# Moving the flags of the second routing's counts to the stationary side, with 16-bit digits and a state per token

## The chip, the cores and the metric

One NeuronCore of a Trainium2 chip runs the whole program. The metric is the device time in microseconds (us) of one execution. In the rows, PE is TensorE's matmuls, PEld its loads of the stationary operand, DVE is VectorE, ACT is ScalarE, POOL is GpSimd, and SP is SyncE, which issues transfers.

## The reference

The program computes attention, then a mixture of experts with free routing (MoE 1), then a second one with limited places (MoE 2). The change lies mostly in MoE 2:

```python
def _moe2_ref(x, w_gate, w1, w2):
    N, D = x.shape            # 3072, 512
    E = w_gate.shape[1]       # 8; w1[e] is 512 x 1024, w2[e] 1024 x 512
    cap = N // E              # 384 places per expert
    flat = (x @ w_gate).flatten()
    order = np.argsort(-flat)
    assigned = -np.ones(N); counts = np.zeros(E)
    for idx in order:                        # best score first
        tok, e = idx // E, idx % E
        if assigned[tok] >= 0 or counts[e] >= cap:
            continue
        assigned[tok] = e; counts[e] += 1
    ...
    for e in range(E):
        h = np.maximum(x[assigned == e] @ w1[e], 0.0)
        out[assigned == e] = h @ w2[e]
```

## The kernel before

The kernel has three stages in time: attention to about 225 us, MoE 1 to about 389 us, MoE 2 to the end. Tokens lie as 128 partitions by NT = 24 columns.

**MoE 1** runs 10 tiles of 128 tokens. In each, TensorE makes the hidden layer in two halves (L1017), ScalarE applies the relu to each half (L1289), and TensorE multiplies by the second matrix (L1032) once both halves are there.

**MoE 2, the routing.** The greedy loop of the reference is replaced by E - 1 = 7 phases and a last list. A phase k takes each free token's best open expert (`first_best`, L1460 to L1464, the best score in `value`, the expert as a one-hot `cand_h`) and finds the score at which the first expert is full. It finds that score's 32 bits in six rounds of 4, 4, 6, 6, 6 and 6 bits. A round r has 15 or 63 candidate digits, made into float thresholds by integer operations on `key`. VectorE compares all values with them into `reach` (L1672, two halves of 12 columns). TensorE counts per expert and threshold (L1065, 24 matmuls with `cand_h[:, j, :]`, 8 columns, stationary and 63 flags moving). VectorE compares the counts with the room left (L1682), TensorE spreads the flags over the partitions (L1070), VectorE counts the flags to get the digit (L1686) and updates `key`. Then follow ties, the list of the tokens and its transfer (L1074, L1049, L1050, L1085). In all a phase has 16 TensorE steps, numbered n = 0 to 15: 2r and 2r+1 are the two of round r, 12 is L1074, 13 and 14 are L1049 with L1050 (12 after the sums of L1708, 13 and 14 after the scans of L1610), 15 is L1085 (one-hot rows made by L1629).

**MoE 2, the experts.** TensorE, expert by expert: 32 "up" products (L1124, 8 blocks f of 4; the trace shows each product as two instructions), relu of each block on ScalarE (L1309), and 24 "down" products (L1137, 3 row blocks c of 8). The steps of the routing are written between these products by `expert2`: `product(units)` adds 3 for an up product and 4 for a down product, and step n is written when the sum reaches its number in `spacing`. While expert i runs, the steps AHEAD to 15 of phase i+1 come first, and then the steps 0 to AHEAD-1 of phase i+2. Steps 0 to 15 of phase 0 and 0 to AHEAD-1 of phase 1 run before the first expert, when TensorE has nothing else. After 18 of the 24 down products `turn2` transposes the next expert's tokens (L1097), which POOL has gathered by indirect transfers (L810) from the list.

```python
            AHEAD = 4
            UP, DOWN = 3, 4
            TURN_AT = CT * FC - 6
            spacing = [18, 7, 8, 7] + [12, 8] * (ROUNDS - 2) + [15, 11, 8, 17]
```

Order is set by these hand-written queues and by semaphores; `plink` makes each dependent VectorE instruction wait for the one before.

## Time and profile before

| | us |
|---|---|
| median of 3 runs | 870.46 (867.44 to 872.6) |
| the profiled execution's own time | 868.02 |
| its span, first to last instruction | 865.7 |
| TensorE busy in the span | 756.2 (87%) |
| VectorE busy | 375.1 (43%) |

The profiled execution's time is 2.3 us above its span, and 2.4 us below the median of the runs. The page cuts the span into 40 slices, and gives the busy share in each and the granted clock of TensorE, whose two levels are 1.2 and 2.4 GHz.

### The profile page before, as it was taken

What the parts mean: (1) busy time and instruction counts of PE and PEld (TensorE: products, weight loads), DVE (VectorE), ACT (ScalarE), POOL (GpSimd) and SP (SyncE); (2) the same over time, 40 slices, a digit from 0 to 9 for tenths busy, and PEclk for the clock granted to TensorE, in tenths of its full rate; (3) what the DMA queues carried; (4) which work ended last, traced back from release to release, by engine and by line L of the source; (5) the groups of instructions that cost most, each with busy time, mean ns of one, the idle gap of its engine ahead of it and who ended that gap; (6) DMA issues with size and microseconds to landing.
All of it is one profiled execution on the core that took longest, in us unless ns stands there. A gap on an engine that the chain in (4) does not pass through costs nothing.

```text
span 865.7 us, 14421 instructions
## 1 busy us (share of the span) xinstructions
PE 756.2 (87%) x4750; PEld 514.1 (59%) x4750; DVE 375.1 (43%) x1532; ACT 221.0 (26%) x685; POOL 189.9 (22%) x251
## 2 busy tenths in 40 slices
PE   3888989995699999992269999999999999999996
PEld 2788989995568778661135454454544545445552
DVE  3576777786111121125735537355473554700000
ACT  3667787881001111110011111111101111011110
POOL 8364646440111111111010200202002020121101
PEclk9799999996699999995559999999999999999998
DMA  9899986687743369000240703306042060453000
GB/s 222 183 196 218 214 204 148 154 245 281 271 165 109 138 221 390 21 4 6 93 140 0 256 14 142 126 0 256 12 159 109 0 257 13 173 190 137 37 0 37
DMA packets 130468, 119.91 MB, mean 139 GB/s; under 512 B 95858, under 2 KB 95858, under 8 KB 130224
## 3 DMA queue, kind: packets, MB, share of 16 engines
q1 hardware_dynamic: 118192, 88.45, 33.9%
q10 hardware_dynamic: 6464, 14.73, 5.5%
q0 software_dynamic: 5760, 16.03, 5.1%
q8 instruction: 33, 0.54, 0.3%
q14 instruction: 19, 0.16, 0.1%
HBM read 105.95 MB, written 16.50 MB: 141 GB/s over the span
## 4 chain that ended last, share of the span: by engine, by line
PE 76%; DVE 10%; issue 5%; DMA 3%; SPq 3%; ACT 1%; POOL 1%; ACTq 0%; POOLq 0%; another core or an unknown queue 0%; DVEq 0%
PE bank L1124 21%; PE bank L1137 18%; PE bank L1017 9%; PE bank L1032 8%; PE bank L1065 4%; PE bank L877 3%; PE bank L898 3%; PE bank L920 2%; PE bank L887 1%; SPq L466 1%; PE bank L1097 1%; DVE scratch L1347 1%; PE bank L997 1%; DVE shared L1358 1%; PE bank L1070 1%
## 5 line engine op out<-in xcount | busy, mean ns | idle before, releaser
L1124 PE MATMUL bank<-scratch,weights 128*128 128x384 f32 x512 | 182.3, 501 | 0.7 <-ACT scratch L1303 0.7
L1137 PE MATMUL bank<-weights,scratch 128*128 128x512 f32 x384 | 176.9, 604 | 4.9 <-issue 2.5
L1124 PEld LDWEIGHTS bank<-scratch,weights 128*128 128x128 f32 x512 | 94.1, 191 | 61.5 <-issue 5.2
L1137 PEld LDWEIGHTS bank<-weights,scratch 128*128 128x128 f32 x384 | 68.5, 190 | 74.5 <-issue 72.0
L1206 ACT ACTIVATE scratch<-shared,neg_max 128x120 f32<-128x120 f32 x192 | 73.4, 383 | 33.5 <-DVE neg_max L1358 20.9
L1309 ACT ACTIVATE scratch<-bank 128x384 f32<-128x384 f32 x64 | 31.5, 492 | 169.9 <-PE bank L1124 169.9
L665 POOL TENSOR_TENSOR scratch<-scratch,row_inv 128x480 f32<-128x480 f32 x48 | 47.4, 988 | 79.8 <-DVE row_inv L1368 79.6
L1017 PEld LDWEIGHTS bank<-mix,weights 128*128 128x128 f32 x512 | 61.2, 197 | 5.1 <-issue 5.1
L1017 PE MATMUL bank<-mix,weights 128*128 128x128 f32 x512 | 62.1, 280 | 1.4 <-DVE mix L1572 1.4
L807 POOL COPY idx<-token_list 128x3 int32 (+1 forms) x8 | 1.5, 186 | 263.6 <-DVE token_list L1645 257.2
L1032 PE MATMUL bank<-weights,mix 128*128 128x512 f32 x128 | 58.4, 599 | 0.0
L1315 ACT COPY scratch<-bank 128x512 f32<-128x512 f32 x24 | 14.1, 587 | 165.0 <-PE bank L1137 165.0
L877 PE MATMUL bank<-scratch 128*128 128x120 f32 x384 | 54.3, 288 | 2.0 <-POOL scratch L657 2.0
L1358 DVE CUSTOM_DVE_ANT_0 shared<-bank,scratch 128x120 f32<-128x120 f32 x192 | 42.7, 279 | 29.4 <-PE bank L877 29.3
L1672 DVE TENSOR_TENSOR mix<-mix 128x756 bf16<-128x756 f32 (+1 forms) x70 | 54.7, 823 | 1.2
L898 PE MATMUL bank<-shared,mix 120*128 120x128 f32 x384 | 51.2, 276 | 4.2 <-issue 2.3
L822 POOL DMA_INDIRECT out<-scratch,idx x24 | 23.8, 990 | 138.3 <-ACT scratch L1315 136.5
L1065 PEld LDWEIGHTS bank<-mix 128*8 128x8 bf16 x1008 | 32.9, 88 | 31.5 <-DVE mix L1672 27.5
L877 PEld LDWEIGHTS bank<-scratch 128*128 128x128 f32 x384 | 48.9, 200 | 2.4 <-POOL scratch L657 2.4
L898 PEld LDWEIGHTS bank<-shared,mix 120*128 120x128 f32 x384 | 47.1, 193 | 4.7 <-issue 2.5
L1065 PE MATMUL bank<-mix 128*8 128x63 bf16 (+1 forms) x1008 | 39.1, 190 | 12.2 <-DVE mix L1672 12.0
L1682 DVE TENSOR_SCALAR mix<-bank,mix 8x63 bf16<-8x63 f32 (+1 forms) x42 | 10.8, 257 | 72.6 <-PE bank L1065 70.6
(230 smaller groups left out, 950.4 us busy)
## 6 DMA issues: line engine op xcount, KB each, us to landing
weights<-in_moe_w SPq DMA_DIRECT2D x20, 2048.0 KB, 8.0
scratch<-in_moe_w SPq DMA_DIRECT2D x8, 2048.0 KB, 15.8
weights<-in_moe_w ACTq DMA_DIRECT2D x16, 512.0 KB, 6.2
mix<-in_v SPq DMA_DIRECT2D x40, 192.0 KB
rows<-row SPq DMA_DIRECT2D x24, 264.5 KB, 3.5
weights<-in_k SPq DMA_DIRECT2D x24, 256.0 KB, 4.9
scratch<-in_q SPq DMA_DIRECT2D x24, 256.0 KB, 4.3
weights<-in_v ACTq DMA_DIRECT2D x24, 192.0 KB, 3.9
```

The lines of the kernel that those rows point to most:

```text
L665: nc.gpsimd.tensor_tensor(out=x, in0=x, in1=inv, op=ALU.mult).then_inc(s.p_scaled, 1)
L877: last = mm(sc[g % 2][:, h * W:(h + 1) * W], qbd[g // 2 % 2][:, h, g % 2, :], kwin[b % 2][:, h, n, :], start=True, stop=True)
L898: last = mm(ob[g % 2][:, h * P:(h + 1) * P], vwin[g % VR][0:W, h * P:(h + 1) * P], pT[g % 2][0:W, h * P:(h + 1) * P], start=True, stop=True)
L1017: last = mm(o, w1_sb[at_][:, c, f * P:(f + 1) * P], xT1[:, c, :], start=(c == 0), stop=(c == C - 1), skip_group_check=True)
L1032: last = mm(yb[:, :], hT1[:, f, :], w2_sb[at_][:, f, :], start=(f == 0), stop=(f == FC - 1))
L1065: last = mm(counts[0:E, 0:ROUND_KEYS[r]], cand_h[:, j, :], reach[:, j, 0:ROUND_KEYS[r]], start=(j == 0), stop=(j == NT - 1), skip_group_ch ...
L1124: last = mm(hb2[f % 2][:, 0:CAP], w1_sb[odd][:, c, f * P:(f + 1) * P], xT2[odd][:, c, :], start=(c == 0), stop=(c == C - 1), skip_group_ch ...
L1137: last = mm(yb2[c % 2][:, :], hT2[odd][:, f, c * P:(c + 1) * P], w2_sb[odd][:, f, :], start=(f == 0), stop=(f == FC - 1), skip_group_check ...
L1206: a.activation(probs[g % PR][:, h, :], masked[g % 2][:, h, :], ACT.Exp, bias=neg_max[:, g % 2, h:h + 1], scale=-1.0, accum_out=row_sum[:, ...
L1309: a.activation(hT2[odd][:, f, :], bank[3 + f % 2][:, 0:CAP], ACT.Relu).then_inc(s.hidden2_s, 1)
L1358: v_.tensor_tensor_reduce(masked[g % 2][:, h, :], bank[g % 2][:, h * W:(h + 1) * W], m, -SCALE, FAR, ALU.add, ALU.min, neg_max[:, g % 2, h ...
L1672: v_.tensor_tensor(out=reach[:, a_:b_, 0:wide_r], in0=value[:, a_:b_].rearrange("p (j o) -> p j o", o=1).to_broadcast(shape), in1=keys.bit ...
```

## The change

The counts change sides: `reach`, the flags of 15 or 63 keys, becomes the stationary operand and `cand_h` with 8 columns the moving one, so that the counts lie as keys by experts. The room of each expert can then be compared in place (the matmul L1063, its semaphore `told` and a copy go), and the sum step spreads 8 columns instead of 63. The key is no longer built as a number: after round 0 each token's score is cut into six digits in 16-bit floats, and a `state_h` per token holds its next digit, or something beyond the range if the token has already fallen above or below. Rounds 1 to 5 compare that state with a constant row of keys, both 16-bit, in pairs of columns. AHEAD becomes 6. The wait for the relu is split, in MoE 2 (the eighth block is awaited only before the eighth product) and in MoE 1 (the second half before the fifth). A few copies of 8 columns become an addition of 0.0.

```diff
-        reach = apart(NT, KEYS, dt=BF16)
-        thresholds = apart(KEYS, dt=I32)
-        key = apart(1, dt=I32)
-        sign = apart(1, dt=I32)
+        reach = apart(NT // 2, KEYS, 2, dt=BF16)
+        sign_i = apart(NT, dt=I32)
+        order_i = apart(NT, dt=I32)
+        digits_i = apart(len(BITS), NT, dt=I32)
+        digits_h = apart(len(BITS), NT, dt=BF16)
+        state_h = apart(NT, dt=BF16)
+        alive_h = apart(NT, dt=BF16)
+        past_h = apart(NT, dt=BF16)
         digit = apart(1)
-        digit_i = apart(1, dt=I32)
-        enough = apart(KEYS)
-        enough_h = apart(KEYS + 1, dt=BF16)
-        remain_col = apart(1)
+        enough_h = apart(E, dt=BF16)
         above = apart(2 * NT, dt=BF16)
         both_n = apart(2 * E, dt=BF16)
...
-                const(nc.gpsimd.iota(digit_row[:, :], pattern=[[1, KEYS]], base=1, channel_multiplier=0))
+                const(nc.gpsimd.iota(digit_row[:, :], pattern=[[1, ROUND_KEYS[0]]], base=1, channel_multiplier=0))
+                const(nc.gpsimd.iota(iota_keys[:, :, :], pattern=[[1, KEYS], [0, 2]], base=1, channel_multiplier=0,
+                                     allow_small_or_imprecise_dtypes=True))
...
-                        pe.wait_ge(s.hidden_made, CREDIT + 2 * g + 2)
+                        pe.wait_ge(s.hidden_made, CREDIT + 2 * g + 1)
                         for f in range(FC):
+                            if f == FC // 2:
+                                pe.wait_ge(s.hidden_made, CREDIT + 2 * g + 2)
                             if f == FC - 2:
                                 pe.wait_ge(s.gathered, 16 * (g + 2))
                                 turn1()
...
                             pe.wait_ge(s.judged, 3 * ROUNDS * k + 3 * r + 1 + j // (NT // 2))
-                        if n == 0 and j == 0:
-                            pe.sem_inc(s.waits_apart, 1)
-
-                            mm(tot[0:E, 0:1], room_e[0:1, :], ones_f[0:1, 0:1], start=True, stop=True,
-                               skip_group_check=True).then_inc(s.told, 1)
-                        last = mm(counts[0:E, 0:ROUND_KEYS[r]], cand_h[:, j, :], reach[:, j, 0:ROUND_KEYS[r]],
+                        last = mm(counts[0:ROUND_KEYS[r], 0:E], reach[:, j // 2, 0:ROUND_KEYS[r], j % 2], cand_h[:, j, :],
                                   start=(j == 0), stop=(j == NT - 1), skip_group_check=True)
                     last.then_inc(s.counted, 1)
                 elif n < 2 * ROUNDS:
                     pe.wait_ge(s.judged, 3 * ROUNDS * k + 3 * r + 3)
-                    mm(counts[:, 64:64 + ROUND_KEYS[r]], ones[0:E, :], enough_h[0:E, 0:ROUND_KEYS[r]], start=True, stop=True,
+                    mm(counts[:, 64:64 + E], ones[0:ROUND_KEYS[r], :], enough_h[0:ROUND_KEYS[r], :], start=True, stop=True,
...
-            AHEAD = 4
+            AHEAD = 6
...
             spacing = [18, 7, 8, 7] + [12, 8] * (ROUNDS - 2) + [15, 11, 8, 17]
...
-                pe.wait_ge(s.hidden2_s, CREDIT + FC * (i + 1))
+                pe.wait_ge(s.hidden2_s, CREDIT + FC * i + FC - 1)
                 for c in range(CT):
 
                     pe.wait_ge(s.y2_s, CREDIT + CT * i + (1 if c == 2 else 0))
                     for f in range(FC):
+                        if c == 0 and f == FC - 1:
+                            pe.wait_ge(s.hidden2_s, CREDIT + FC * (i + 1))
...
                 lg = bank[7][:, 0:NL]
-                v_.tensor_copy(row[t % 2][:, 0:E], lg[:, 0:E])
+                v_.tensor_scalar(row[t % 2][:, 0:E], lg[:, 0:E], 0.0, None, ALU.add)
...
-                link(v_.tensor_scalar(digits_at[r], digit_row[:, 0:ROUND_KEYS[r]], SHIFTS[r], None, ALU.logical_shift_left))
-
+            link(v_.tensor_scalar(first_digits[:, :], digit_row[:, :], SHIFTS[0], None, ALU.logical_shift_left))
             half = ROUND_KEYS[0] // 2
-            v_.tensor_scalar(first_keys[:, 0:half], digits_at[0][:, 0:half], -1, None, ALU.bitwise_xor)
-            link(v_.tensor_scalar(first_keys[:, half:], digits_at[0][:, half:], -(1 << 31), None, ALU.bitwise_xor))
+            v_.tensor_scalar(first_keys[:, 0:half], first_digits[:, 0:half], -1, None, ALU.bitwise_xor)
+            link(v_.tensor_scalar(first_keys[:, half:], first_digits[:, half:], -(1 << 31), None, ALU.bitwise_xor))
             dve.wait_ge(s.scores_in, 16)
 
             ROUNDS = len(BITS)
@@ -1658,47 +1655,47 @@
                 first_best(plink, scores2, value, hot, cand_h)
                 for r in range(ROUNDS):
                     wide_r = ROUND_KEYS[r]
-                    flags = counts[:, 64:64 + wide_r]
-                    keys = first_keys[:, :] if r == 0 else thresholds[:, 0:wide_r]
-                    if r == 1:
-                        plink(v_.tensor_scalar(keys, digits_at[r], key, None, ALU.bitwise_xor))
-                    elif r:
-
-                        plink(v_.tensor_scalar(keys, digits_at[r], key, digit_i, ALU.bitwise_xor,
-                                               ALU.bitwise_xor))
-
-                    for a_, b_ in ((0, NT // 2), (NT // 2, NT)):
-                        shape = [P, b_ - a_, wide_r]
-                        v_.tensor_tensor(out=reach[:, a_:b_, 0:wide_r],
-                                         in0=value[:, a_:b_].rearrange("p (j o) -> p j o", o=1).to_broadcast(shape),
-                                         in1=keys.bitcast(F32).rearrange("p (o k) -> p o k", o=1).to_broadcast(shape),
-                                         op=ALU.is_ge).then_inc(s.judged, 1)
+                    state = digits_h[:, 0, :] if r == 0 else state_h
+                    for a_, b_ in ((0, NT // 4), (NT // 4, NT // 2)):
+                        shape = [P, b_ - a_, wide_r, 2]
+                        if r == 0:
+                            ins = v_.tensor_tensor(
+                                out=reach[:, a_:b_, 0:wide_r, :],
+                                in0=value[:, 2 * a_:2 * b_].rearrange("p (j o s) -> p j o s", o=1, s=2).to_broadcast(shape),
+                                in1=first_keys[:, :].bitcast(F32).rearrange("p (o k u) -> p o k u", o=1, u=1).to_broadcast(shape),
+                                op=ALU.is_ge)
+                        else:
+                            ins = v_.tensor_tensor(
+                                out=reach[:, a_:b_, 0:wide_r, :],
+                                in0=iota_keys[:, 0:wide_r, :].rearrange("p (o k) s -> p o k s", o=1).to_broadcast(shape),
+                                in1=state[:, 2 * a_:2 * b_].rearrange("p (j o s) -> p j o s", o=1, s=2).to_broadcast(shape),
+                                op=ALU.is_le)
+                        ins.then_inc(s.judged, 1)
                     if r == 0:
-                        dve.wait_ge(s.told, ph + 1)
-                        plink(v_.tensor_copy(remain_col[0:E], tot[0:E, 0:1]))
-                    elif r > 1:
-                        plink(v_.tensor_tensor(out=key, in0=key, in1=digit_i, op=ALU.bitwise_xor))
+                        plink(v_.tensor_scalar(sign_i, value.bitcast(I32), 31, -(1 << 31), ALU.arith_shift_right,
+                                               ALU.bitwise_or))
+                        plink(v_.tensor_tensor(out=order_i, in0=value.bitcast(I32), in1=sign_i, op=ALU.bitwise_xor))
+                        for i in range(ROUNDS):
+                            ins = v_.tensor_scalar(digits_i[:, i, :], order_i, SHIFTS[i], ROUND_KEYS[i],
+                                                   ALU.logical_shift_right, ALU.bitwise_and)
+                        plink(ins)
+                        v_.tensor_copy(digits_h[:, 0, :], digits_i[:, 0, :])
+                        plink(v_.tensor_scalar(digits_h[:, 1:, :], digits_i[:, 1:, :], 1.0, None, ALU.add))
                     dve.wait_ge(s.counted, 2 * ROUNDS * ph + 2 * r + 1)
-                    v_.tensor_scalar(enough_h[0:E, 0:wide_r], counts[0:E, 0:wide_r], remain_col[0:E], None,
-                                     ALU.is_ge).then_inc(s.judged, 1)
+                    v_.tensor_tensor(out=enough_h[0:wide_r, :], in0=counts[0:wide_r, 0:E], in1=room_e[0:wide_r, :],
+                                     op=ALU.is_ge).then_inc(s.judged, 1)
                     dve.wait_ge(s.counted, 2 * ROUNDS * ph + 2 * r + 2)
-
-                    plink(v_.tensor_scalar(enough[:, 0:wide_r], flags, 0.5, 0.0, ALU.is_gt, ALU.add, accum_out=digit))
-                    shift = SHIFTS[r]
-                    if r == 0:
-                        plink(v_.tensor_copy(digit_i, digit))
-                        plink(v_.tensor_scalar(key, digit_i, shift, None, ALU.logical_shift_left))
-                        plink(v_.tensor_scalar(sign, key, 31, -1, ALU.arith_shift_right, ALU.bitwise_xor))
-                        plink(v_.tensor_scalar(sign, sign, -(1 << 31), None, ALU.bitwise_or))
-                        plink(v_.tensor_tensor(out=key, in0=key, in1=sign, op=ALU.bitwise_xor))
-                    else:
-                        plink(v_.tensor_scalar(digit_i, digit, float(1 << shift), None, ALU.mult))
-                plink(v_.tensor_tensor(out=key, in0=key, in1=digit_i, op=ALU.bitwise_xor))
-
-                closing = key.bitcast(F32)
-                v_.tensor_scalar(above[:, 0:NT], value, closing, None, ALU.is_gt)
-                v_.tensor_scalar(above[:, NT:], value, closing, None, ALU.is_ge)
-                plink(v_.tensor_scalar(equal_t, value, closing, None, ALU.is_equal))
+                    plink(v_.tensor_reduce(digit, counts[:, 64:64 + E], AX, ALU.max))
```

The first place is TensorE's queue at the end of an expert's up products and the start of its down products (`product` steps 12 to 15). Before:

```order
L1124 MATMUL bank<-scratch,weights 128x384 x3
L1073 ISA
L1074 MATMUL bank<-mix,ones 128x16 [waits totals_done]
L1130 ISA [waits w2_in0]
L1133 ISA [waits hidden2_s]
L1137 MATMUL bank<-weights,scratch 128x512 [waits y2_s]
L1137 MATMUL bank<-weights,scratch 128x512 x2
L1077 REGISTER_ALU
L1049 MATMUL bank<-mix,before 128x24 [waits totals_done]
L1050 MATMUL bank<-mix,ones 128x23
L1137 MATMUL bank<-weights,scratch 128x512 x2
L1049 MATMUL bank<-mix,before 128x24 [waits mine_ready]
```

And now (line numbers of the changed kernel; L1121 is the up product, L1136 the down product):

```order
L1071 MATMUL bank<-mix,ones 128x16 [waits totals_done]
L1121 MATMUL bank<-scratch,weights 128x384 x3
L1119 REGISTER_ALU
L1121 MATMUL bank<-scratch,weights 128x384 [waits hidden2_s]
L1074 REGISTER_ALU
L1051 MATMUL bank<-mix,before 128x24 [waits totals_done]
L1052 MATMUL bank<-mix,ones 128x23
L1121 MATMUL bank<-scratch,weights 128x384 x3
L1051 MATMUL bank<-mix,before 128x24 [waits mine_ready]
L1052 MATMUL bank<-mix,ones 128x23
L1127 REGISTER_ALU [waits w2_in1]
L1136 MATMUL bank<-weights,scratch 128x512 [waits y2_s,hidden2_s]
```

Steps 12, 13 and 14 now stand among the up products; the wait of `hidden2_s` at the first L1136 is for seven blocks, that for the eighth comes later (not shown). Between step 12 and the second L1051 stand 7 up products; before it was 5 down products and the full relu wait.

The second place is TensorE's queue in front of the first expert (steps of phase 1, then `turn2`). Before:

```order
L1085 MATMUL bank<-mix 128x6 x24
L1063 MATMUL bank<-ones_f,mix 8x1
L1065 MATMUL bank<-mix 8x15 x24
L1070 MATMUL bank<-mix,ones 128x15
L1065 MATMUL bank<-mix 8x15 x24
L1070 MATMUL bank<-mix,ones 128x15
L1097 MATMUL bank<-ident,scratch 128x128 x12
```

And now:

```order
L1082 MATMUL bank<-mix 128x6 x24
L1062 MATMUL bank<-mix 15x8 x24
L1067 MATMUL bank<-mix,ones 128x8
L1062 MATMUL bank<-mix 15x8 x24
L1067 MATMUL bank<-mix,ones 128x8
L1062 MATMUL bank<-mix 63x8 x24
L1067 MATMUL bank<-mix,ones 128x8
L1094 MATMUL bank<-ident,scratch 128x128 x12
```

A third round of phase 1, the first with 63 keys, has moved in front of the first expert.

## Rows read from the trace of the kernel before

**Rows 1.** The page's head: span, busy time of each engine.
```profile
span 865.7 us, 14421 instructions
PE 756.2 (87%) x4750; PEld 514.1 (59%) x4750; DVE 375.1 (43%) x1532; ACT 221.0 (26%) x685; POOL 189.9 (22%) x251
```
**Rows 2.** Windows: stretch, its us, busy by engine, clock, DMA.
```profile
390.00:442.00 52.00, 12.68 (x232) 9.65 (x232) 33.30 (x126) 0.00 (x0) 5.54 (x7) 0.50 0.21 59
500.00:740.00 240.00, 234.07 (x1381) 123.19 (x1380) 118.95 (x424) 32.98 (x63) 26.09 (x29) 1.00 0.26 98
```
**Rows 3.** Timeline of PE in the second expert: start, us, what.
```profile
508.12 2.85 PE L1124 MATMUL bank<-scratch,weights 128*128 128x384 f32 x8
510.90 0.92 PE L1065 MATMUL bank<-mix 128*8 128x63 bf16 x24
511.74 2.20 PE L1124 MATMUL bank<-scratch,weights 128*128 128x384 f32 x6
513.88 0.20 PE L1070 MATMUL bank<-mix,ones 8*128 8x63 bf16 x1
514.01 2.85 PE L1124 MATMUL bank<-scratch,weights 128*128 128x384 f32 x8
```
**Rows 4.** The same timeline, from up to down products.
```profile
528.49 0.17 PE L1074 MATMUL bank<-mix,ones 128*128 128x16 bf16 x1
529.24 2.84 PE L1137 MATMUL bank<-weights,scratch 128*128 128x512 f32 x6 [0.57 <-ACT scratch L1309]
533.77 0.18 PE L1049 MATMUL bank<-mix,before 128*128 128x24 bf16 x1
```
**Rows 5.** Timeline of PE, last expert, which has no steps.
```profile
814.84 20.86 PE L1124 MATMUL bank<-scratch,weights 128*128 128x384 f32 x64
836.32 20.84 PE L1137 MATMUL bank<-weights,scratch 128*128 128x512 f32 x48 [0.63 <-issue]
```
**Rows 6.** Timeline of DVE after step 12 of that phase.
```profile
528.73 0.17 DVE L1714 TENSOR_TENSOR mix<-mix,bank 128x8 f32<-128x8 f32 x1 [0.82 <-PE bank L1074]
533.38 0.21 DVE L1610 TENSOR_TENSOR_SCAN mix<-mix 128x24 bf16<-128x24 bf16 x1
```
**Rows 7.** Timeline of PE: 8 moving columns in MoE 1.
```profile
298.27 0.96 PE L997 MATMUL bank<-gate_weights,mix 128*128 128x8 f32 x8
299.12 5.42 PE L1032 MATMUL bank<-weights,mix 128*128 128x512 f32 x12
```
**Rows 8.** Timeline of PE, end of the sixth expert.
```profile
752.08 0.78 PE L1085 MATMUL bank<-mix 128*128 128x6 bf16 x24
752.72 1.96 PE L1137 MATMUL bank<-weights,scratch 128*128 128x512 f32 x4
759.72 2.82 PE L1137 MATMUL bank<-weights,scratch 128*128 128x512 f32 x6
763.93 1.09 PE L1097 MATMUL bank<-ident,scratch 128*128 128x128 f32 x8 [1.39 <-DMA scratch<-rows,idx]
```
**Rows 9.** Timeline of PE, rounds 0 and 1 of phase 2.
```profile
491.17 0.18 PE L1070 MATMUL bank<-mix,ones 8*128 8x15 bf16 x1 [0.44 <-issue]
493.44 0.75 PE L1065 MATMUL bank<-mix 128*8 128x15 bf16 x24 [0.18 <-DVE mix L1672]
```
**Rows 10.** Timeline of DVE, phase 0, a 63-key round and L1629.
```profile
404.68 1.80 DVE L1672 TENSOR_TENSOR mix<-mix 128x756 bf16<-128x756 f32 x2
407.38 0.27 DVE L1682 TENSOR_SCALAR mix<-bank,mix 8x63 bf16<-8x63 f32 x1 [0.83 <-PE bank L1065]
408.78 1.80 DVE L1672 TENSOR_TENSOR mix<-mix 128x756 bf16<-128x756 f32 x2
429.19 1.76 DVE L1629 TENSOR_TENSOR mix<-iota_pair,mix 128x3072 bf16<-128x3072 bf16 x1
```
**Rows 11.** Timeline of PE at the lower clock, phases 0 and 1.
```profile
431.50 0.88 PE L1085 MATMUL bank<-mix 128*128 128x6 bf16 x24 [3.14 <-DVE mix L1638]
442.16 2.91 PE L1097 MATMUL bank<-ident,scratch 128*128 128x128 f32 x12
```

25 lines of the change are left out of this document (15 added, 10 removed).

## Prediction, made before the changed kernel ran

> **What bounds the kernel now.** I began with the page's head: TensorE is busy for 756 of 866 us [rows 1]. The windows show where it is not. From 500 to 740 us it is busy 234 of 240 us at the full clock, VectorE only half [rows 2]: there every instruction put into TensorE's queue costs its time, and VectorE's work costs nothing unless TensorE arrives before it. From 390 to 442 us it is the other way round: TensorE is busy 12.7 of 52 us at 1.2 GHz, VectorE 33 [rows 2]. So I price the change twice: by TensorE's queue in the loops, by the length of the dependent chain in front of the first expert. Attention and MoE 1 hardly move: in MoE 1 the down products follow at once on the 8 gate matmuls [rows 7], so the split wait there removes nothing, and I take it at 0.
>
> **The relu wait.** Step 12 starts at 528.49, the first down product at 529.24, and the page names the relu [rows 4]. Without the wait L1074 would hold the queue for some 0.05, so 0.7 is saved in each of six experts. In the last one 64 up instructions take 20.86 with a tail of 0.49, a pitch of 0.323; the down products could start at 835.53 and do at 836.32: 0.8, in two experts [rows 5]. Block seven is done long before, block eight (0.5 of relu) has seven products of 0.85 as cover. Sum -5.8.
>
> What is late next is VectorE. It needs from step 12 (528.49) to the end of its second scan (533.38 + 0.21) 5.1, with 0.05 for the signal 5.15 [rows 4, 6]. Before, TensorE reached the second L1049 at 5.28 after step 12, just behind. Now seven up products (7 x 0.647 = 4.53) and two or three insertions (0.13 each; eight up instructions before L1065 take 2.78 in place of 2.59 [rows 3]) make 4.8. TensorE waits 0.35 at step 14, in six experts: +2.1. Queued behind it are the expert's down products, which ScalarE's copies and POOL's scatters then get later. Step 15 then has four products (3.4) against VectorE's unchanged 3.3, as before.
>
> **The counts.** 24 of them, 8 columns stationary and 63 moving, hold the queue from 510.90 to 511.74, 0.84 [rows 3]. After it 63 columns are stationary and 8 move. The trace has no such load; the bounds are two rows with 128 stationary columns. The 32-bit ones of L997, 8 columns moving, take 299.12 - 298.27 = 0.85 for 8, 0.106 each, 0.83 ns a column [rows 7]; 63 columns by that are 0.052, 24 of them 1.26, with 0.1 for handing over to the next product 1.35: +0.5 a round. The 16-bit ones of L1085 take 752.72 - 752.08 = 0.64 for 24 [rows 8]: -0.2 a round. I take the first. Half the bytes of L997's would make L1085's loads twice as quick; they are four times as quick, 0.21 ns a column. So something beyond width helps the full 128 columns of 16 bits, and nothing in the trace says that 63 columns have it. This is where I chose, and it decides the case. 23 rounds of 63 keys remain among the products (24 before: four each in phases 1 to 6): +11.5. Rounds of 15 keys have loads of 0.0125 by either price, under their pitch of some 0.03: no change.
>
> The Trainium skill, TensorE: Matmul & The Clock Gate, section Weight-path perf modes — Fast Weight Load (FWL) and DoubleRow, says that the fast load is on only with exactly 128 weights and a type other than fp32. By its section on LDWEIGHTS a plain load takes the columns over 1.2, 52.5 ns for 63. The trace's two rates fit it (0.106 and 0.027 for 128 columns); that it holds for 63 no row shows. By the rule the counts cost what I take, by L1085's row 16 us less.
>
> **The sum step** moves 8 in place of 63 columns: at 2.4 GHz 0.023 less, 23 times, -0.5. **The moved round.** One full round (count and sum step) leaves the queue of the loops: 514.01 - 508.12 less 14 x 0.323, 1.4: -1.4. **Waits in rounds 0 and 1.** At round 1 TensorE waits 0.18 for the flags [rows 9]; VectorE's key update and threshold (five small operations) shrink to three, with two products as cover: gone, five times, -0.9. The 0.44 before round 0's sum step [rows 9] I leave as it is: L1063 goes, but six digits and their conversion come before VectorE's comparison, about 1.5 by the rows of small operations (0.2 a dependent link). Bounds: -2.2, and +2 if that chain ends after the counts.
>
> **The last gather.** In the sixth expert TensorE could turn at 759.72 + 6 x 0.427 = 762.3 and does at 763.93, waiting for the gather [rows 8]. The list is now written 20 units, five down products or 4.3, earlier: -1.6. The gather of expert 1 before the loop is hidden too.
>
> **In front of the first expert.** A 63-key round takes 408.78 - 404.68 = 4.10: 2.70 from flags to comparison, 1.40 from there to the next flags [rows 10]. The 16-bit flags in pairs run like L1629, 3072 elements in 1.76 [rows 10], so 756 in about 0.55 in place of 0.9; TensorE can start at 0.6 and needs 1.35 and its end: 2.2 in place of 2.7. The second part stays about 1.35, three links on 24 columns in place of threshold and key. With the lost key operations at the end phase 0 is 2.8 shorter, and so are the list and the gather; phase 1's own rounds give 0.2. But the third round of phase 1 now stands before `turn2`, at 442.16 until now [rows 11]: 1.0 to make the state, 2.2, 0.3 for the sum step: +3.5. Net +0.5. The round no longer hides behind up products there.
>
> The small copies turned additions and the set-up (one shift for six) lie beside transfers: 0.
>
> **Sum:** -5.8 + 2.1 + 11.5 - 0.5 - 1.4 - 0.9 - 1.6 + 0.5 = +3.9 on the profiled 868.0: 871.9. The median of the runs shown is 2.4 higher, so 874.
>
> **Rivals.**
> *Cheap loads* (chance 0.15). 63 columns load at L1085's rate. Then counts give 23 x -0.2 = -4.6, and each of the five serial rounds is 0.65 shorter, -2.8 in place of +0.5 at the start: -15.5, 855. For it: L1085 reads the same 16-bit layout, with a step of two. Against it: the reasons above. The skill's rule speaks against it.
> *Half-hidden loads* (0.13). A load overlaps more with the array's work, pitch about 0.045: +0.25 a round: 23 x 0.25 = 5.8 in place of 11.5, start -0.5: -2.8, 867.5. For it: in rows 3 all of a count's 8-column load is already out of sight.
> *Slower by the lower clock* (0.12). The loads before the first expert might take twice as long at 1.2 GHz: 2.5 in place of 1.26 for a count, in five serial rounds (four of phase 0, one of phase 1): +6.2, 880.5. It decides from 0.055 us a load up. Against it: L1085 takes 0.88 there and 0.64 at the full clock [rows 8, 11], 1.4 times, not 2.
> *My forecast* (0.6), own range 869 to 879, from +0.3 to +0.6 a count and the bounds of round 0.
>
> **Chances.** A measurement of this kernel can tell about 0.5%, 4.4 us. My forecast lies at +3.9, so of its 0.6 I give 0.36 to no change and 0.24 to slower; cheap loads are faster; half-hidden ones are split evenly; the lower clock is slower. Faster 0.15 + 0.07 = 0.22, same 0.36 + 0.06 = 0.42, slower 0.24 + 0.12 = 0.36. The range 862 to 880 leaves out cheap loads and the end of the last rival.
>
> **What would show it.** In the profile after: L1062 with 63 keys, 24 of them from first start to the next product 1.35 (cheap: 0.65); no ACT wait before the first L1136, but some 0.35 before the second L1051; an expert with its steps about 1.4 longer than before; `turn2`'s first L1094 near 442.7 with no gather wait; no wait for the gather in the sixth expert; the flags on VectorE at 0.55. Wrong would make me above all the price of a 63-column load; next a VectorE chain in round 0 that ends after the counts, or a wait at step 14 larger than reckoned.

## The result, and the profile after

The changed kernel takes 867.0 us (median of 20 runs, 858.9 to 871.5) where the kernel before takes 871.2 (20 runs, 867.1 to 875.3). The ratio is 0.9948, with a 95% interval of 0.9927 to 0.9969: about 3 to 6 us faster. I had forecast 874, no change or slower. The span of the profiled execution falls from 865.7 to 860.1, its own time from 868.0 to 865.4: after the change 5.3 lie outside the span, where 2.3 did before. Most other executions have 2.3, and nothing in the profile tells where the rest went. Two executions of later runs, of 2672 and 1571 us where the others of their kernels took about 855 and 859, are left out of medians and ratios; what held them up isn't known.

The profiled execution of the changed kernel is shorter than most. The 20 runs have spans from 856.6 to 869.2 with a median of 864.6, and mean granted clocks from 0.946 to 0.933 with a median of 0.9375; the longer ones tend to have the lower clock. The profiled one has 860.1 and 0.942. The granted clock has two levels, so these numbers give some 108 us at 1.2 GHz for the median run and 100 for the profiled one. By my estimate that is worth up to 4 of the 4.5 us between them, half of the 8, as far as TensorE is the bound in those stretches. The run with four steps ahead, below, shows where such a stretch can lie.

The head of the page after and its row of the granted clock, then the windows that answer to [rows 2]:

```profile
span 860.1 us, 14325 instructions
PE 752.6 (88%) x4736; PEld 516.2 (60%) x4736; DVE 347.3 (40%) x1513; ACT 220.9 (26%) x685; POOL 190.6 (22%) x251
...
PEclk9799999997699999996569999999999999999999
```
```profile
390.00:442.00 52.00, 13.05 (x241) 11.17 (x242) 30.98 (x136) 0.00 (x1) 5.65 (x8) 0.52 0.22 62
500.00:740.00 240.00, 233.21 (x1353) 124.07 (x1353) 102.79 (x425) 33.43 (x64) 26.43 (x29) 1.00 0.26 98
```

Over the whole span VectorE has lost 28 us of work and TensorE 3.6. In the loops TensorE is the bound as before: 233 of 240 us.

The timeline of TensorE in the second expert answers to [rows 3] and [rows 4]: start, us, what, and in brackets the idle time and who ended it.

```profile
501.10 2.75 PE L1121 MATMUL bank<-scratch,weights 128*128 128x384 f32 x8
503.78 0.94 PE L1062 MATMUL bank<-mix 128*63 128x8 bf16 x24
504.65 2.21 PE L1121 MATMUL bank<-scratch,weights 128*128 128x384 f32 x6
506.80 0.18 PE L1067 MATMUL bank<-mix,ones 63*128 63x8 bf16 x1
506.90 2.85 PE L1121 MATMUL bank<-scratch,weights 128*128 128x384 f32 x8
...
526.52 0.19 PE L1051 MATMUL bank<-mix,before 128*128 128x24 bf16 x1 [0.20 <-DVE mix L1607]
526.56 0.17 PE L1052 MATMUL bank<-mix,ones 128*128 128x23 bf16 x1
526.73 3.67 PE L1136 MATMUL bank<-weights,scratch 128*128 128x512 f32 x8
```

Four things can be read here. 24 counts hold TensorE's queue from 503.78 to 504.65: 0.87, where they held it 0.84 before [rows 3]. I had forecast 1.35. The sum step holds it 0.10 in place of 0.13. The first down product no longer waits for ScalarE [rows 4]. Step 14 waits 0.20 for VectorE. An expert with its steps takes 53.85 in place of 53.67, where I had said about 1.4 longer.

Round 0 of the next phase, on all three engines (it answers to [rows 9], one phase on). POOL's L810 issues the gathers of the next expert's rows, L822 a scatter of results:

```profile
534.12 0.60 DVE L1662 TENSOR_TENSOR mix<-mix,first_keys 128x180 bf16<-128x180 f32 x2
535.07 0.59 DVE L1679 TENSOR_SCALAR mix<-mix 128x24 int32<-128x24 int32 x6
535.77 0.21 DVE L1683 TENSOR_SCALAR mix<-mix 128x120 bf16<-128x120 int32 x1
538.21 0.15 DVE L1685 TENSOR_TENSOR mix<-bank,mix 15x8 bf16<-15x8 f32 x1 [2.22 <-remote]
...
535.34 0.75 PE L1062 MATMUL bank<-mix 128*15 128x8 bf16 x24
536.02 1.13 PE L1136 MATMUL bank<-weights,scratch 128*128 128x512 f32 x2
538.42 0.17 PE L1067 MATMUL bank<-mix,ones 15*128 15x8 bf16 x1 [1.27 <-issue]
...
534.55 1.05 POOL L810 DMA_INDIRECT scratch<-rows,idx  x1 [0.31 <-issue]
535.91 1.00 POOL L810 DMA_INDIRECT scratch<-rows,idx  x1 [0.30 <-issue]
537.21 1.01 POOL L822 DMA_INDIRECT out<-scratch,idx  x1 [0.30 <-issue]
```

VectorE's digits end at 535.98 and the last count starts at 535.93, but the comparison of the counts starts only at 538.21, 2.3 later. TensorE then waits 1.27 before the sum step, where it waited 0.44 before. In the rounds after this one the comparison comes 0.20 behind the last count. The trace also has the time of the semaphore's update, the signal itself: it comes 2.25 behind the start of the last count, and the comparison starts 0.03 after it. In the rounds after this one it comes after 0.18 or 0.19. So VectorE is not what is late. It is the signal, or the counts behind it, since the profile only models the ends of matmuls. There is a new cost of 0.8 in five phases that no term of my sum has.

The sixth expert (against [rows 8]) no longer waits for its gather, and waits 0.77 for VectorE once, as before:

```profile
748.88 0.19 PE L1051 MATMUL bank<-mix,before 128*128 128x24 bf16 x1 [0.77 <-DVE mix L1607]
...
753.10 7.11 PE L1136 MATMUL bank<-weights,scratch 128*128 128x512 f32 x16
760.05 1.04 PE L1094 MATMUL bank<-ident,scratch 128*128 128x128 f32 x8
```

A 63-key round of phase 0 on VectorE and TensorE (against [rows 10]) takes 410.32 - 406.95 = 3.37 in place of 4.10. The flags take 1.01 for both halves and 24 counts at 1.2 GHz 1.45. In round 0 of that phase the comparison starts 1.01 behind the last count, where it started 0.21 behind it before: the digits stand ahead of it and nothing covers them. No term of my sum has that either.

```profile
406.95 1.01 DVE L1668 TENSOR_TENSOR mix<-iota_keys,mix 128x756 bf16<-128x756 bf16 x2
409.04 0.16 DVE L1685 TENSOR_TENSOR mix<-bank,mix 63x8 bf16<-63x8 f32 x1 [1.08 <-PE bank L1062]
410.32 1.02 DVE L1668 TENSOR_TENSOR mix<-iota_keys,mix 128x756 bf16<-128x756 bf16 x2
...
407.56 1.45 PE L1062 MATMUL bank<-mix 128*63 128x8 bf16 x24 [1.49 <-DVE mix L1668]
```

Where the time went, from the starts of single instructions (an expert runs from its first up product to the next one's). The last two columns are profiles of the same two kernels on another chip, which come in below:

```
                                  before   after  | before   after (chip D)
start of VectorE's phase 0        396.93  399.35  | 400.88  400.68
from there to the first expert     48.81   47.86  |  47.68   47.08
first expert                       56.58   53.89  |  55.04   54.81
second to fifth expert            214.72  215.37  | 211.73  210.08
sixth                              53.85   50.50  |  52.24   50.50
seventh                            43.93   43.06  |  43.93   43.06
eighth, to the end                 50.90   50.04  |  50.90   50.04
```

Two of these rows are no effect of the change. The 2.4 ahead of phase 0 come with attention: MoE 1's first hidden product already starts at 225.03 before and 227.66 after. In the first expert the clock rises to 2.4 GHz at 451.5 before, 5.8 into the expert, and at 447.0 after, at its start; on chip D it rises at 452.5 before and 452.2 after, and the expert differs by 0.23. The rest of the gain is in the last three experts. The four in the middle, which carry 16 of the 23 rounds of 63 keys, lose 0.65 here and gain 1.65 on chip D.

### The profile page after: what moved, and what is told of

Its sections match the earlier page's. It is cut to its first block, busy times and chain, and to the rows that moved or that the text cites. A ratio compares the mean times of both kernels' runs of the same rounds, so it can differ in the third digit from the quotient of the medians.

```text
span 860.1 us, 14325 instructions
## 1 busy us (share of the span) xinstructions
PE 752.6 (88%) x4736; PEld 516.2 (60%) x4736; DVE 347.3 (40%) x1513; ACT 220.9 (26%) x685; POOL 190.6 (22%) x251
## 4 chain that ended last, share of the span: by engine, by line
PE 73%; DVE 13%; issue 4%; SPq 3%; DMA 2%; POOL 1%; ACT 1%; ACTq 0%; another core or an unknown queue 0%; POOLq 0%; DVEq 0%
PE bank L1136 18%; PE bank L1121 17%; PE bank L1017 9%; PE bank L1034 8%; PE bank L1062 4%; PE bank L877 3%; PE bank L898 3%; PE bank L920 2%; PE bank L887 2%; SPq L465 1%; PE bank L1094 1%; DVE scratch L1346 1%; PE bank L997 1%; DVE shared L1357 1%; PE bank L864 1%
## 5 line engine op out<-in xcount | busy, mean ns | idle before, releaser
L1121 PE MATMUL bank<-scratch,weights 128*128 128x384 f32 x512 | 178.0, 495 | 0.7 <-ACT scratch L1302 0.7
L1136 PE MATMUL bank<-weights,scratch 128*128 128x512 f32 x384 | 177.7, 603 | 0.0
L1121 PEld LDWEIGHTS bank<-scratch,weights 128*128 128x128 f32 x512 | 93.0, 189 | 60.0 <-issue 4.7
L1136 PEld LDWEIGHTS bank<-weights,scratch 128*128 128x128 f32 x384 | 68.8, 190 | 67.9 <-issue 66.5
L1062 PEld LDWEIGHTS bank<-mix 128*63 128x63 bf16 (+1 forms) x1008 | 35.6, 110 | 46.3 <-DVE mix L1662 18.5
L822 POOL DMA_INDIRECT out<-scratch,idx x24 | 23.7, 989 | 169.9 <-ACT scratch L1314 168.1
L1062 PE MATMUL bank<-mix 128*63 128x8 bf16 (+1 forms) x1008 | 39.4, 174 | 24.3 <-DVE mix L1662 14.5
L1685 DVE TENSOR_TENSOR mix<-bank,mix 63x8 bf16<-63x8 f32 (+1 forms) x42 | 6.6, 156 | 90.4 <-PE bank L1062 78.5
L1034 PEld LDWEIGHTS bank<-weights,mix 128*128 128x128 f32 x128 | 23.1, 190 | 23.0 <-issue 23.0
```

The source lines that it names most:

```text
L822: nc.gpsimd.indirect_dma_start(out=out, out_offset=bass.IndirectOffsetOnAxis(ap=idx2[odd][:, c:c + 1].bitcast(U32), axis=0), in_=y2[odd][: ...
L1034: last = mm(yb[:, :], hT1[:, f, :], w2_sb[at_][:, f, :], start=(f == 0), stop=(f == FC - 1))
L1062: last = mm(counts[0:ROUND_KEYS[r], 0:E], reach[:, j // 2, 0:ROUND_KEYS[r], j % 2], cand_h[:, j, :], start=(j == 0), stop=(j == NT - 1), s ...
L1121: last = mm(hb2[f % 2][:, 0:CAP], w1_sb[odd][:, c, f * P:(f + 1) * P], xT2[odd][:, c, :], start=(c == 0), stop=(c == C - 1), skip_group_ch ...
L1136: last = mm(yb2[c % 2][:, :], hT2[odd][:, f, c * P:(c + 1) * P], w2_sb[odd][:, f, :], start=(f == 0), stop=(f == FC - 1), skip_group_check ...
```

## The experiments

The chips are called A (first four kernels), B, C and D. Each ratio is against the kernel before on the same chip.

**What each part gives** (chip A, before 868.0). The changed kernel itself was not run unaltered on chips A, B and C, so where a run is set against it, that is its profile or its ratio from the result.

The waits alone (in MoE 1 the second half of the relu is awaited singly as well):
```diff
-pe.wait_ge(s.hidden2_s, CREDIT + FC * (i + 1))
+pe.wait_ge(s.hidden2_s, CREDIT + FC * i + FC - 1)
 ...
+    if c == 0 and f == FC - 1:
+        pe.wait_ge(s.hidden2_s, CREDIT + FC * (i + 1))
```


> The kernel before with nothing but the relu waits split (the last relu block awaited singly, in MoE 1 the second half singly). Theory A (the relu wait is what the change gains, and the counts with 63 stationary columns cost about nothing): 0.7 to 0.8 saved in eight experts, 0.2 to 0.35 given back at step 14 in six, so -4 to -5 us against before, ratio 0.9945 to 0.9955, as fast as the whole change. Rival B (the gain is VectorE's shorter chain, and a late VectorE takes over whatever the relu wait leaves): within 1.5 us of before.

Measured 866.0, ratio 0.997 (0.9946 to 0.9993): -2.0 by the medians, -2.6 by the ratio, between the two. The two last experts gave 0.87 each. In an expert with steps the period went from 53.67 to 53.54, because step 14 took up most of what the relu left:

```profile
589.27 0.19 PE L1051 MATMUL bank<-mix,before 128*128 128x24 bf16 x1 [0.45 <-DVE mix L1614]
```

The digits alone (AHEAD = 4 and the old waits in the changed kernel).


> The changed kernel with the old relu waits and four steps ahead: only the digits, the state and the flags as weights are left of the change. Theory A: the counts give +0.7 in all, the sum step -0.5, round 1 -0.9, phase 0 about -3, and the sum step of round 0, which in the changed kernel waits 1.27 in place of 0.45, +4 over five phases: the sum is within 1.5 us of before, 870 to 872.5. Rival B: faster than before by 3 to 5 us, since the gain lies here. My forecast on record, were its price of the loads right: +8 to +11 us.

867.5, ratio 0.9984 (0.996 to 1.0007), within 1 us of before; by the forecast's price of the loads it would have been at 876 to 879. The period was 54.05, with the relu wait of 0.57 to 0.65 and one of 1.17 to 1.24 in round 0.

```diff
-AHEAD = 6
+AHEAD = 4
```


> The changed kernel with four steps ahead in place of six, all else kept. Theory A: the round that leaves the queue of the loops (-1.4) and the gather of the last expert (-1.4) come back, the third round of phase 1 before the first expert (3.2 to 3.5 at the lower clock) goes: within 1 us of the changed kernel. Rival C (the earlier list and gather are the gain of the change): 3 us or more slower than the changed kernel.

866.6, ratio 0.9974 (0.9947 to 1.0). From VectorE's phase 0 to the first expert it took 44.45 in place of 47.86, the sixth expert 52.13 in place of 50.50. So six steps ahead cost 3.4 in front of the first expert, at the lower clock, and return 1.6 in the sixth; between four and six the median can't tell. By the ratios the waits alone give 0.3%, the digits alone 0.2% with 1 in the interval, and the whole change gave 0.5%: no single part carries the gain.

This profile shows something else. Twice, at 545.7 and at 654.9, the granted clock falls to 1.2 GHz among the experts, and is back at 549.1 and 658.3. These two experts take 55.32 and 55.30, the one between them 53.96. The fall comes 0.6 after the end of round 0's wait:

```profile
545.10 0.17 PE L1067 MATMUL bank<-mix,ones 15*128 15x8 bf16 x1 [1.25 <-DVE mix L1685]
545.20 3.32 PE L1136 MATMUL bank<-weights,scratch 128*128 128x512 f32 x4
```
```profile
545.80:549.00 3.20, 3.20 (x26) 1.18 (x25) 0.70 (x4) 0.59 (x1) 0.65 (x1) 0.50 0.26 104
```

The same is in two profiles of chip B: in that of the single loads, whose kernel is the changed one up to its end, at 596.0 and 705.3 (those experts take 55.53, their neighbours 53.87 and 53.80), and in that with POOL held, at 699.8, in the one expert of the last with a wait of 1.13. All five falls begin within 0.7 of the end of a round 0 wait of 1.1 to 1.3; of the 19 waits that long in the profiles, 14 have none behind them. No profile of the kernel before or of its variants, and none on chips C and D, has one among the experts. So a late signal may cost 1.3 to 1.7 beyond its wait, which the profile after, without such a fall, doesn't show. That the wait brings the fall about, and that the lower mean clocks among the 20 runs come from such falls, no run tested.

The kernel before with `AHEAD = 6`.


> The kernel before with six steps ahead and nothing else. Theory A: -1.4 for the moved round, -1.6 for the last gather, and +4.1 for a serial 63-key round of the old kind before the first expert: +1, 871 to 873. Rival C: faster than before by 3 us or more.

874.2, ratio 1.0065 (1.0038 to 1.0092): +6, more than either. With the old 4.1 round the chain ahead of the first expert grows by 4.0, the period by 0.4 (round 0's wait becomes 0.91, and step 14 waits 0.20 with 0.25 of the relu left behind it), and the sixth expert returns 3.3. That makes 2.4 with the four experts in the middle; phase 0 also started 3.2 later in this profile than in that of the kernel before, which is no effect of the edit, and the rest of the 6 I can't place. With the old round six ahead loses 6; with the new one the medians show no loss.

**What a load costs.** Behind the last down product of the changed kernel 24 matmuls of each kind ran, back to back (chip B).
```diff
+for w in (8, 15, 32, 48, 63, 64, 96, 127, 128):
+    for _ in range(24):
+        mm(bank[3][0:w, 0:8], ones[:, 0:w], cand_h[:, 0, :], start=True, stop=True)
 ... (stationary columns with a step of two; 8 with 15, 63, 126 moving; 32 bits)
```


> The changed kernel with extra matmuls behind the last down product, 24 back to back of each kind: 8, 15, 32, 48, 63, 64, 96, 127 and 128 stationary columns of 16 bits with 8 moving; 15, 32 and 63 stationary columns taken with a step of two; 8 stationary columns with 15, 63 and 126 moving; 8, 32, 63 and 128 stationary columns of 32 bits with 8 moving. My forecast on record: 0.052 each for 63 columns of 16 bits, 0.106 for 128 of 32 bits, 0.027 for 128 of 16. Theory L (from the changed kernel's rows): 0.030 to 0.036 for 63 columns of 16 bits whatever the step, near 0.03 for all narrower ones, and growing above 64 if the fast load needs all 128 columns, staying near 0.03 if it doesn't.

Windows of it: us, matmuls (about five of them already under way at the left edge), loads, other engines, and the granted clock as the third number from the end. In order: 63 and 64 columns; 64; 127; 128; then 32-bit, 32 columns and 128 columns.

```profile
861.30:862.20 0.90, 0.90 (x33) 0.90 (x32) 0.00 (x0) 0.00 (x0) 0.00 (x0) 1.00 0.74 291
862.35:862.85 0.50, 0.50 (x14) 0.50 (x12) 0.00 (x0) 0.00 (x0) 0.00 (x0) 0.50 0.15 33
865.10:867.30 2.20, 2.20 (x23) 2.20 (x22) 0.00 (x0) 0.00 (x0) 0.00 (x0) 0.50 0.00 0
867.55:868.15 0.60, 0.60 (x25) 0.60 (x25) 0.00 (x0) 0.00 (x0) 0.00 (x0) 0.50 0.00 0
876.60:877.60 1.00, 1.00 (x37) 1.00 (x35) 0.00 (x0) 0.00 (x0) 0.00 (x0) 1.00 0.00 0
883.00:892.00 9.00, 9.00 (x44) 9.00 (x43) 0.00 (x0) 0.00 (x0) 0.00 (x0) 0.50 0.00 0
```

The clock fell to 1.2 GHz at 862.3, in the middle of the kinds. From start to start, by the single records (the profile has two instructions for each 32-bit matmul, and these are times of one instruction; the 106 at 2.4 GHz is that of rows 7):

```
stationary columns, type      2.4 GHz   1.2 GHz
8 to 48,  16 bits               25 ns
63 or 64, 16 bits               32        53    (63 taken with a step of two: 54)
96        16 bits                         81
127       16 bits                        107
128       16 bits                         27
8 / 32    32 bits               25 / 32
63        32 bits               58       107
128       32 bits    106 [rows 7]        213
8, with 63 / 126 moving, 16 bits          52 / 104
```

Beyond 48 columns, a column of 16 bits costs 0.5 ns at the full clock (63 and 64 columns; wider ones ran only at the lower clock) and 0.84 at the lower one; of 32 bits 0.8 to 0.9 and 1.7. My 0.83 was the 32-bit price at the full clock. The type alone makes most of the factor of two that I had written down and set aside: 1.8 for 63 columns at the full clock (58 against 32), 2.0 at the lower one (107 against 53).

In place, each 63-key count issued twice (chip C, the same edit in both kernels):
```diff
+for twice in range(2 if r > 1 else 1):
     last = mm(counts[...], ...)
```


> The kernel before with each of the 24 count matmuls of every 63-key round issued twice (the first time into columns that nobody reads). It prices a count of the old form (8 stationary columns of 16 bits, 63 moving) in place: 24 rounds of 63 keys run among the products, four in front of the first expert. Expected 24 times about 0.033, 0.8 a round, so +3.2 an expert where TensorE is the bound and about +22 us in all.

> The changed kernel with each count of every 63-key round issued twice in the same way: the price of the new form (63 stationary columns, 8 moving) in place. The price of my forecast on record, 0.052 each: 1.25 a round, +5 an expert. The price that the run of single loads gave at the full clock, 0.032: 0.77 a round, +3.1 an expert, within 0.1 of the old form. So the difference of the two doubled kernels tells what the change of sides costs a round: +0.5 by the forecast, 0.0 by the loads.

Ratios 1.0236 (1.0208 to 1.0263) and 1.0206 (1.0177 to 1.0236). 48 counts of the old form, then of the new:

```profile
565.85 1.62 PE L1066 MATMUL bank<-mix 128*8 128x63 bf16 x48
567.39 2.21 PE L1126 MATMUL bank<-scratch,weights 128*128 128x384 f32 x6
```
```profile
572.33 1.73 PE L1063 MATMUL bank<-mix 128*63 128x8 bf16 x48
574.00 2.21 PE L1123 MATMUL bank<-scratch,weights 128*128 128x384 f32 x6
```

The 24 further ones cost 1.54 - 0.84 = 0.70 and 1.67 - 0.87 = 0.80, 29 and 33 ns each. At the full clock the change of sides costs +0.03 to +0.10 a round, not +0.5.

**The late signal of round 0** (chip B, before 869.8).

POOL holds its gathers until round 0 is counted, in the first four experts:
```diff
+if held:
+    wait_apart(pool, s.counted, 2 * ROUNDS * (e + 1) + 1)
 for c in range(CT):
     nc.gpsimd.indirect_dma_start(
```


> The changed kernel, but GpSimd starts the three gathers of an expert's rows only after TensorE has signalled the 24 counts of round 0 of the running phase (in four experts of the loop; the last two as they were). Theory P (the signal of the counts arrives late because GpSimd is issuing gathers at the time: it comes 2.2 after the last count with gathers beside it, 0.2 in rounds without): VectorE's comparison comes within 0.3 of the counts, TensorE's wait of 1.2 before the sum step of round 0 is gone in those experts, the gather is still in time, so -3 to -5 us against the changed kernel. Rival D (the comparison is late for VectorE's digits or for something on TensorE itself): the wait stays at 1.2, the time is the changed kernel's.

859.4, ratio 0.988 (0.9849 to 0.9911), the period 52.54. The comparison came at 539.68, 0.2 behind the last count, and the wait was gone. In round 1, beside which the gathers now ran, it came 1.65 late, where more products cover it:

```profile
538.89 0.75 PE L1066 MATMUL bank<-mix 128*15 128x8 bf16 x24
539.68 0.15 DVE L1689 TENSOR_TENSOR mix<-bank,mix 15x8 bf16<-15x8 f32 x1
...
541.92 1.05 POOL L812 DMA_INDIRECT scratch<-rows,idx  x1 [0.31 <-issue]
542.65 0.75 PE L1066 MATMUL bank<-mix 128*15 128x8 bf16 x24
543.27 1.00 POOL L812 DMA_INDIRECT scratch<-rows,idx  x1 [0.31 <-issue]
544.89 0.15 DVE L1689 TENSOR_TENSOR mix<-bank,mix 15x8 bf16<-15x8 f32 x1 [2.64 <-PE bank L1066]
545.25 0.17 PE L1071 MATMUL bank<-mix,ones 15*128 15x8 bf16 x1
```

The digits behind the comparison:
```diff
                     ins.then_inc(s.judged, 1)
-                    if r == 0: ... (sign, order, digits)
                     dve.wait_ge(s.counted, 2 * ROUNDS * ph + 2 * r + 1)
                     v_.tensor_tensor(out=enough_h..., op=ALU.is_ge)
+                    if r == 0: ... (sign, order, digits)
                     dve.wait_ge(s.counted, 2 * ROUNDS * ph + 2 * r + 2)
```


> The changed kernel with the sign, order and digit operations of round 0 (about 1.5 of VectorE) moved behind the comparison of the counts, beside the wait for the sum step. Rival D: the comparison of round 0 starts up to 1 earlier and the wait of 1.2 at the sum step goes back to the 0.45 of the kernel before: -4 us. Theory P: the comparison waits for the signal as before, the digits then come behind it and are hidden by the products before round 1 only in part: within 1 us in the loops; 0.8 is saved once in phase 0 and once in phase 1, where nothing else delays it.

863.7, ratio 0.9937 (0.9908 to 0.9965). The comparison came 1.43 to 1.6 behind the count in place of 2.2 to 2.4, as in the kernel before (1.4), and the period fell by 0.35 to 53.5. 0.39 of what the sum step gained came back as a wait for round 1's flags. In front of the first expert it cost 1.3 more. So both theories hold a part: beside the gathers the signal is late by 1.4 anyway, and by 2.2 where the digits run in between, though the digits had ended before. But the digits aren't needed for a later signal: in the kernel before with six steps ahead, where GpSimd issues its gathers 0.3 earlier against the counts, it came after 1.85. What makes the signal late I can't say.

More products between the counts and the sum step:
```diff
-spacing = [18, 7, 8, 7] + ...
+spacing = [18, 18, 8, 7] + ...
```


> The changed kernel with 18 in place of 7 units between the counts and the sum step of round 0, so that two more down products stand between them. Theory: whatever makes the comparison late, 1.7 of products cover the 1.2 of waiting: the expert's period falls from 53.85 to 52.65, five experts, -6 us, 860 to 863, if nothing else becomes late (later steps move back by two products; the last of them still lies before the expert ends). Rival E: another wait takes its place (round 1's flags, the rows of the next expert), and less than 2 us are won.

858.1, ratio 0.9864 (0.9828 to 0.9901), some 12 us below the kernel before. The period was 52.5, where 52.65 was expected, with no new wait. The signal was still 2.2 to 2.35 late; the products covered it.

Two more on chip C, where the kernel before took 863.2: the same spacing in the kernel before, and in the changed kernel with 12 in place of 8 units ahead of step 14 besides.


> The kernel before with 18 in place of 7 units between the counts and the sum step of round 0. It tells how much of what the spacing gained in the changed kernel could be had without the change: the wait of 0.45 at the sum step goes, perhaps the 0.17 at round 1's counts too, so the period of an expert falls from 53.69 to 53.1 to 53.25 and the whole by 2 to 3.5 us.

> The changed kernel with 18 units ahead of round 0's sum step and 12 in place of 8 ahead of step 14 (the sum along the tokens for the list). The wait of 0.19 at step 14 goes and a product more stands there; everything behind it moves back one product. Period 52.55 to 52.35, another -1 us over the spaced kernel, unless the list, one product later, makes the gather late in the sixth expert (+0.4 once).

The kernel before gained nothing from the spacing (863.2, ratio 1.0001, 0.9984 to 1.0018), and waited 0.97 for a gather of rows in its second expert, which it doesn't in its old order. The other took 854.6, ratio 0.9886 (0.9858 to 0.9913). In all four profiles of this chip the comparison of round 0 comes 0.2 to 0.3 behind the counts among the experts: there was no late signal to cover.

**Kernel or chip** (chip D, before 863.0). Both kernels unaltered, and both spacings.


> The changed kernel unaltered, on one chip with the three that follow. If the late signal belongs to the chip: a chip that shows it gives a wait of 1.2 at round 0's sum step, a period of 53.8 and a ratio near 0.995; a chip that doesn't gives no such wait, a period of 52.6 and, since the kernel before loses its 0.45 there too, a ratio of 0.990 to 0.993. If it belongs to the kernel: the wait of 1.2 shows on this chip whatever the other three do.

> The kernel before unaltered, ratio 1. If the lateness belongs to the chip, it has the waits of 0.45 and 0.17 in rounds 0 and 1 exactly where the changed kernel has its 1.2 on this chip, and a period of 53.7; else none of them and 53.05.

> The changed kernel with 18 units ahead of round 0's sum step and 12 ahead of step 14. Its products cover even a signal that is 2.2 late, so its period is 52.0 to 52.4 on either kind of chip: ratio 0.982 to 0.985 on a chip with late signals, 0.987 to 0.990 on one without.

> The changed kernel with 18 units ahead of round 0's sum step alone. Against the one with 12 at step 14 it prices that edit on one chip: period 52.54 against 51.99 (0.19 of it is the wait at step 14), so 2 to 3 us slower than it.

The changed kernel 858.0, ratio 0.9935 (0.9912 to 0.9959); the kernel before against itself 1.0015 (0.9996 to 1.0033); with both spacings 854.3, ratio 0.9888 (0.986 to 0.9916); with the first alone 858.7, ratio 0.9961 (0.9941 to 0.9981). So where the signal is prompt the first spacing gains nothing (858.0 without it), and the second is worth 4.4, where I had expected 2 to 3. The changed kernel in round 0 on this chip, with the same instructions at the same distances as in the profile above:

```profile
536.80 0.75 PE L1062 MATMUL bank<-mix 128*15 128x8 bf16 x24
537.37 1.00 POOL L810 DMA_INDIRECT scratch<-rows,idx  x1 [0.30 <-issue]
537.59 0.15 DVE L1685 TENSOR_TENSOR mix<-bank,mix 15x8 bf16<-15x8 f32 x1
538.54 0.17 PE L1067 MATMUL bank<-mix,ones 15*128 15x8 bf16 x1
538.67 1.01 POOL L822 DMA_INDIRECT out<-scratch,idx  x1 [0.30 <-issue]
```

So the late signal belongs to the chip, or to something that differs between the jobs: it is in all profiles of A and B and in the first two of the study, and in none of the eight of C and D. Without it the fourth expert takes 52.91 before and 52.55 after, and 51.99 with both spacings (windows of chip D, in this order; the second number is TensorE's busy time):

```profile
609.49:662.40 52.91, 52.10 (x306) 27.29 (x305) 27.37 (x99) 7.35 (x14) 6.29 (x7) 1.00 0.30 110
```
```profile
607.65:660.20 52.55, 52.11 (x304) 27.52 (x303) 23.54 (x97) 7.35 (x14) 6.38 (x7) 1.00 0.30 110
```
```profile
606.60:658.59 51.99, 51.75 (x305) 27.52 (x303) 23.54 (x98) 7.36 (x14) 6.38 (x7) 1.00 0.30 111
```

TensorE's busy time is the same before and after, 52.10 and 52.11: four rounds of counts with their sides exchanged, and six sum steps, come out even. The 0.36 between the periods is a wait of 0.57 for the relu less one of 0.20 at step 14. The second spacing takes that 0.20 and 0.36 of busy time besides. Most of it lies at the same place: in this expert the six up instructions ahead of step 14 hold the queue 2.39 with the first spacing alone (630.85 to 633.24, the wait in it) and 2.02 with both, and its second matmul, L1052, 0.17 and 0.02. The six instructions are busy for 2.19 in both, but with nothing to wait for the next one starts 0.17 before their end. So the wait of 0.20 cost about 0.5 there. The sixth expert falls from 50.50 to 49.27 as well; its wait of 0.78 at step 14 is gone.

## Why the prediction was wrong

**The step that failed is the price of a count**: "24 of them 1.26, with 0.1 for handing over to the next product 1.35: +0.5 a round", in the sum +11.5. It is 0.87, +0.03 to +0.10 a round, +0.7 to +2.3 in the sum, shown by the profile after, by the single loads and by the doubled counts. The mechanism was right in its first half: columns short of 128 don't load at the rate of 128 (at 1.2 GHz 127 take 107 ns and 128 take 27). So the rival of cheap loads, 0.65 for 24, had the wrong mechanism too, though its price lay as near as that of the half-hidden one (1.09). The second half was wrong: the rate I gave the slow kind was that of 32-bit loads at the full clock, where 63 columns of 16 bits take 32 ns and not 52. In front of the first expert, at 1.2 GHz, they do take 53. The rows of before had both types, but only at 128 columns, where the 16-bit one is the exception; I took the one exception as the reason to drop the factor of two for the type. ("By either price" for 15 keys is a slip too: by the cheap one the load is 0.003. It changes nothing.) The value between the two rows, 63 x 0.83 / 2 = 26 ns and thus hidden or nearly so, stood for no case of mine but the half-hidden rival, at 45 ns. The Trainium skill, TensorE: Matmul & The Clock Gate, sections Weight-path perf modes — Fast Weight Load (FWL) and DoubleRow and LDWEIGHTS (loading the stationary operand), says that the fast load is on with 128 weights and a type other than fp32, and gives the columns over 1.2 as the time of a plain load. The single loads agree on the first (107 ns for 127 columns of 16 bits, 27 for 128, 213 for 128 of 32 bits, all at 1.2 GHz). The second gives 53 for 63 columns, and that is what the run shows at the lower clock; at the full clock, where most counts are, it is 32, and the measurement decides.

With +0.7 in place of +11.5 my sum would have given -6.9, or 863.5 for the median. Between the medians of 20 lie -4.2. What it lacks above all is round 0. The range 862 to 880 holds 867.0, but not by my sum: the counts cost some 10 us less than forecast and round 0 cost 3.9 more.

**Round 0.** "The 0.44 before round 0's sum step [rows 9] I leave as it is", bounds -2.2 and +2: a wait that I carried over without knowing what set its length. On the chips of the recorded profiles it grew to 1.2 to 1.35 in five phases: +3.9, beyond the upper bound, which I had tied to a VectorE chain that ends late. The chain ended in time, and the signal was late. Before the change it was late too, by 1.4, and the 0.44 of [rows 9] came from that. On chips C and D the term is 0, and neither kernel waits there.

**The relu wait**, -5.8: the wait is gone in all eight experts. By the rows it was 0.57 to 0.65 in six and 0.87 in two, -5.2 to -5.6. Right. **Step 14**, +0.35 in six: 0.19 to 0.20, +1.2, and 0.45 with four steps ahead. Right in kind: VectorE's chain took 5.13, as reckoned, but TensorE needed 4.93 in place of 4.8; most of what the split wait frees in an expert with steps was taken up there when it stood alone.

**Sum step** -0.5: 0.13 to 0.10, right. **Moved round and last gather**, -1.4 and -1.6: the sixth expert fell by 3.35, of which the relu less step 14 is 0.43; the rest is 2.9. Right; on chip D, where the kernel before had no wait for that gather, it fell by 1.74. **Round 1**, -0.9: its 0.17 is gone on A and B, and wasn't there on C and D.

**In front of the first expert**, +0.5: measured -0.95 and, on D, -0.6. A 63-key round takes 3.37, I had 3.55; the third round of phase 1 costs 3.4, as said. `turn2` starts 44.3 behind phase 0, 1.0 earlier than before (45.2), where I had it 0.5 later. **The lower clock** as a rival: a 63-column load does take longer there (53 ns against 32), but 24 counts take 1.45, not 2.5, because the price it started from was the wrong one.

The half-hidden rival's 867.5 lies beside the measured 867.0. That is chance: its count cost 0.25 a round, and the real +3.9 of round 0 stood where it had 5.8 for counts.

## What to carry to other kernels

Before a price is carried from one row to another, name each way in which the two differ (columns, type, clock) and look for a pair of rows that differ in one of them alone; where two rows differ by more than the known factor, the odd one is the exception, and it doesn't cancel the factor for the rest. A wait that a program shows beside indirect transfers may be absent on another chip, so a few more products between a signal and the instruction that needs it can be cheap cover: here 18 in place of 7 units left the period at 52.55 where the signal was prompt and were worth 1.3 an expert where it was late, and with four more units at step 14 the kernel had the shortest times of the study, 1.1% below the kernel before on chips C and D. A wait taken away pays in full only where nobody is close behind it: 0.87 in the experts without routing steps, 0.13 in those with them, until the order ahead was changed as well.
